# A block-product layer on one core: layer 2 of the step ahead in two parts, and the x sums after the gates' normalisation

## The reference

```python
def _moe_ref(x, w_gate, w1, w2):          # x: 1152 x 512, E = 8, F = 1024
    logits = x @ w_gate
    P = np.exp(logits - logits.max())
    for _ in range(8):                    # the gates' normalisation
        P /= P.sum(1, keepdims=True) + 1e-09
        P /= P.sum(0, keepdims=True) + 1e-09
        P *= N / E
    out = np.zeros((N, D), dtype=np.float32)
    for e in range(E):
        h = np.maximum(x @ w1[e], 0.0)
        ye = h @ w2[e]
        out += P[:, e:e + 1] * ye
    return out
```

## Time and profile before

| what | value |
|---|---|
| time, median of 3 runs | 1185.52 us (1184.65 to 1187.41) |
| profiled execution: its own time | 1187.6 us |
| profiled execution: span | 1185.8 us |
| PE busy | 1136.4 us (96%), 6974 instructions |
| DVE busy | 749.1 us (63%) |
| ACT busy | 442.9 us (37%) |
| POOL busy | 354.7 us (30%) |
| chain that ended last | PE 81%, DVE 6%, POOL 5%, issue 3%, ACT 3%, DMA 1% |
| mean granted clock of TensorE | 0.983 of full speed |

### The profile page before, as it was taken

The page is one execution under the profiler, slowest core; times in us unless marked ns, Lnnn a source line. Parts: engine busy times, 40 slices in busy tenths (PEclk is TensorE's granted clock), DMA queues, the critical chain, the costliest instruction groups (busy, mean ns, idle before and its releaser), DMA issues.

```text
span 1185.8 us, 19445 instructions
## 1 busy us (share of the span) xinstructions
PE 1136.4 (96%) x6974; PEld 1006.5 (85%) x6979; DVE 749.1 (63%) x1325; ACT 442.9 (37%) x936; POOL 354.7 (30%) x386
## 2 busy tenths in 40 slices
PE   7899798899999999999999999999997999999997
PEld 4678797789899898899888988999896889888885
DVE  5776834775775877776677587561136556665663
ACT  4772122433433443343443343241132334343332
POOL 3332706342333333243333244200001222222221
PEclk8899999999999999999999999999998999999999
DMA  7714001221321221231131121070003666655653
GB/s 177 185 39 147 29 1 53 78 66 36 107 72 36 72 90 51 74 90 36 54 102 48 48 71 36 15 269 28 28 18 112 177 186 179 177 145 162 177 143 80
DMA packets 120775, 109.52 MB, mean 92 GB/s; under 512 B 23712, under 2 KB 95392, under 8 KB 120704
## 3 DMA queue, kind: packets, MB, share of 16 engines
q1 hardware_dynamic: 113624, 93.53, 25.8%
q0 software_dynamic: 5904, 14.75, 5.9%
q10 hardware_dynamic: 1176, 0.30, 0.1%
HBM read 97.64 MB, written 10.91 MB: 92 GB/s over the span
## 4 chain that ended last, share of the span: by engine, by line
PE 81%; DVE 6%; POOL 5%; issue 3%; ACT 3%; DMA 1%; POOLq 0%; DVEq 0%; SPq 0%; ACTq 0%
PE bank L1657 7%; PE bank L1661 6%; PE bank L1659 6%; PE bank L1701 6%; PE bank L1702 6%; PE bank L1703 6%; PE bank L1517 6%; PE bank L1531 6%; PE bank L1518 6%; PE bank L1519 6%; PE bank L1533 6%; PE bank L1532 6%; DVE acc L1200 2%; POOL wopf L614 1%; ACT wop L862 1%
## 5 line engine op out<-in xcount | busy, mean ns | idle before, releaser
L1702 PE MATMUL bank<-w2lo,hS 128*128 128x512 f32 x432 | 168.5, 390 | 0.0
L1701 PE MATMUL bank<-w2hi,hS 128*128 128x512 f32 x432 | 168.5, 390 | 0.0
L1703 PE MATMUL bank<-w2hi,hS 128*128 128x512 f32 x432 | 168.2, 389 | 0.0
L622 POOL TENSOR_TENSOR s<-u,s 128x256 f32<-128x256 f32 (+1 forms) x48 | 38.7, 806 | 346.3 <-DVE u L1220 346.3
L1531 PE MATMUL bank<-w2hi,hhi 128*128 128x512 f32 (+1 forms) x336 | 132.9, 395 | 0.0
L1533 PE MATMUL bank<-w2hi,hlo 128*128 128x512 f32 (+1 forms) x336 | 131.4, 391 | 0.0
L1532 PE MATMUL bank<-w2lo,hhi 128*128 128x512 f32 (+1 forms) x336 | 131.3, 391 | 0.0
L1657 PE MATMUL bank<-xhi,wop 128*128 128x320 f32 (+1 forms) x384 | 115.8, 302 | 5.6 <-ACT s L881 5.6
L1659 PE MATMUL bank<-xlo,wop 128*128 128x320 f32 (+1 forms) x384 | 114.2, 297 | 0.0
L1661 PE MATMUL bank<-xhi,wop 128*128 128x320 f32 (+1 forms) x384 | 114.2, 297 | 0.0
L1025 DVE SCALAR_TENSOR_TENSOR hlo<-bank,hhi 128x336 fp32r<-128x336 f32 (+1 forms) x112 | 58.4, 523 | 70.9 <-ACT hhi L903 40.3
(11 more groups left out here) (259 smaller groups left out, 2759.0 us busy)
## 6 DMA issues: line engine op xcount, KB each, us to landing
w1p<-in_moe_w_dram SPq DMA_DIRECT2D x96, 256.0 KB, 3.5
w1raw<-in_moe_w_dram SPq DMA_DIRECT2D x44, 512.0 KB, 5.4
w2raw<-in_moe_w_dram SPq DMA_DIRECT2D x44, 512.0 KB, 5.4
w2p<-in_moe_w_dram SPq DMA_DIRECT2D x48, 256.0 KB, 2.9
qkraw<-in_q_dram SPq DMA_DIRECT2D x16, 144.0 KB
out_dram<-ysb POOLq DMA_DIRECT2D x3, 768.0 KB, 10.4
x1rows<-acc SPq DMA_DIRECT2D x9, 256.0 KB, 2.0
qkraw<-in_k_dram SPq DMA_DIRECT2D x14, 144.0 KB
```

What stands on the lines that cost most here:

```text
L1701: pe.matmul(y[:, :], hh, w2hi[:, f, :], start=(p == 0 and fi == 0), stop=False)
L1702: pe.matmul(y[:, :], hh, w2lo[:, f, :], start=False, stop=False)
L1703: ins = pe.matmul(y[:, :], hl, w2hi[:, f, :], start=False, stop=(p == POS - 1 and fi == 1))
```

## The change

It has four parts.

1. PE: `products` gets an argument `between`. Behind its third product (S1) PE now runs the first two row tiles of layer 2 of the step before (`FRONT`), and behind the seventh product the other two or three (`BEHIND`).
2. DVE: `weight_lo` is split into two functions, and both halves are for step j+1 instead of j+2. They, and `weight2_lo` (now of step j itself), move from the end of the step to the place between `u2` and `u3`. The additions into `acc` are made in two parts: the first two tiles before `u3`, the others at the end of the step. ACT's and POOL's order for the weights stays.
3. POOL starts `x_sums` only when the first tile of `acc` is written, which is behind the last round of the normalisation.
4. The last x sum of the second block moves: on POOL from before step (1, 0) to behind step (1, 2), on ACT and DVE to the end of step (1, 3), and PE waits for it before the last product of step (1, 4). POOL makes the weight sums of step (1, 0) ahead of the first block's last x sum.

```diff
@@ POOL
+            pool.wait_ge(acc_ready, 1)
             for b in range(2):
                 x_sums(b)
             pool.wait_ge(l1_done, G * FC)
+            weight_sums(1, 0)
             pool.wait_ge(xsum_lo, 6)
             x_last_sum(0)
-            for j in range(2):
-                weight_sums(1, j)
-            x_last_sum(1)
+            weight_sums(1, 1)
             step(1, 0)
             for e in range(1, LAST):
                 for j in range(1, STEPS):
                     step(e, j)
+                    if e == 1 and j == 2:
+                        x_last_sum(1)
                 step(e + 1, 0)
...
+        FRONT, BEHIND, WHOLE_STEP = slice(0, 2), slice(2, None), slice(0, None)
+        def step_tiles(b, part):
+            return range(BLOCKS[b][0] // P, sum(BLOCKS[b]) // P)[part]
@@ ACT, step
                 if (j + 1) % STEPS < POS and not (e == LAST and j == STEPS - 1):
                     weight2_hi(e + (j + 1) // STEPS, (j + 1) % STEPS)
+                if n == POS - 1:
+                    act.wait_ge(xsum_ready, 4)
+                    x_sum_hi(3, 1)
...
             expert(0, 1)
+            weight_hi(1, 0)
             act.wait_ge(xsum_ready, 3)
             x_sum_hi(3, 0)
-            for j in range(2):
-                weight_hi(1, j)
-            act.wait_ge(xsum_ready, 4)
-            x_sum_hi(3, 1)
+            weight_hi(1, 1)
             weight2_hi(1, 0)
             step(1, 0)
@@ DVE, step
                 dve.tensor_tensor(u2_, banks[1][:, 0:h], s1_, ALU.add).then_inc(u2_ready, 1)
+                if j < POS and not first:
+                    weight2_lo(e, j)
+                if not first and not (e == LAST and j == STEPS - 1):
+                    weight_lo(e + (j + 1) // STEPS, (j + 1) % STEPS)
+                    weight_sums_lo(e + (j + 1) // STEPS, (j + 1) % STEPS)
+                if j == POS:
+                    add_tiles(e, 0, FRONT)
+                if j == 0 and not first:
+                    add_tiles(e - 1, 1, FRONT)
                 dve.wait_ge(p7_added, n + 1)
...
                 low(3, s5_)
-                if ahead:
-                    weight_lo(e + (j + 2) // STEPS, (j + 2) % STEPS)
-                if (j + 1) % STEPS < POS and not (e == LAST and j == STEPS - 1):
-                    weight2_lo(e + (j + 1) // STEPS, (j + 1) % STEPS)
+                if n == POS - 1:
+                    x_sum_lo(3, 1)
                 if j == POS:
-                    add_block(e, 0)
+                    add_tiles(e, 0, BEHIND)
                 if j == 0 and not first:
-                    add_block(e - 1, 1)
+                    add_tiles(e - 1, 1, BEHIND)
@@ PE
                 product(S1, t1, banks[2], True, p5_in_bank)
+                if between is not None:
+                    second(*between, FRONT)
                 pe.wait_ge(s1_ready, n + 1)
...
+                if e == 1 and j == POS:
+                    pe.wait_ge(xsum_lo, 8)
                 product(A22, t4, banks[1], False, p4_added)
...
             products(1, 0)
-            pe.wait_ge(xsum_lo, 8)
             for e in range(1, LAST):
                 for j in range(STEPS):
-                    products(e + (j + 1) // STEPS, (j + 1) % STEPS)
-                    second(e, j)
-            for j in range(STEPS):
-                if j + 1 < STEPS:
-                    products(LAST, j + 1)
-                second(LAST, j)
+                    products(e + (j + 1) // STEPS, (j + 1) % STEPS, (e, j))
+                    second(e, j, BEHIND)
+            for j in range(STEPS - 1):
+                products(LAST, j + 1, (LAST, j))
+                second(LAST, j, BEHIND)
+            second(LAST, STEPS - 1)
```

More of the change, by code:

```diff
@@ L1184, in weight_lo, with weight_sums_lo @@
                                   ).then_inc(wop_lo, 1)
+            def weight_sums_lo(e, j):
+                n = e * STEPS + (j - STEPS)
+                hi, lo = (wop[:, j % 2, i, :, :, :] for i in range(2))
                 dve.wait_ge(wop_hi, 2 * n + 2)
@@ L1193, in weight2_lo, with add_tiles @@
                                   ).then_inc(w2s_lo, 1)
-            def add_block(e, b):
-                for i in range(BLOCKS[b][0] // P, sum(BLOCKS[b]) // P):
+            def add_tiles(e, b, part):
+                for i in step_tiles(b, part):
                     dve.wait_ge(l2_done, e * TILES + (i + 1))
@@ L1201, in add_block, with step @@
                                              ALU.mult, ALU.add).then_inc(acc_ready, 1)
-            def step(e, j, ahead=True):
+            def step(e, j):
                 n, h = e * STEPS + (j - STEPS), HALVES[j // POS]
@@ L1266, in group @@
                         if tt == 0:
+                            weight_lo(1, 0)
+                            weight_sums_lo(1, 0)
                             x_sum_lo(3, 0)
-                            weight_lo(1, 0)
                         if tt == 1:
                             weight_lo(1, 1)
-                            x_sum_lo(3, 1)
+                            weight_sums_lo(1, 1)
                     add_tile(e, g * TT + tt, plain)
@@ L1287, in _ @@
             for j in range(1, STEPS):
-                step(LAST, j, j + 2 < STEPS)
+                step(LAST, j)
                 if j == POS + 1:
@@ L1293, in _ @@
             x_back_low(1)
-            add_block(LAST, 1)
+            add_tiles(LAST, 1, WHOLE_STEP)
             for g in range(G):
@@ L1644, in _, with products @@
             group2(0, 0, 2)
-            def products(e, j):
+            def products(e, j, between=None):
                 n, b = e * STEPS + (j - STEPS), j // POS
@@ L1684, in products, with second @@
                     pe.wait_ge(xsum_lo, 7)
+                if e == 1 and j == POS:
+                    pe.wait_ge(xsum_lo, 8)
                 product(A22, t4, banks[1], False, p4_added)
-            def second(e, j):
+            def second(e, j, part=WHOLE_STEP):
                 n, b, p = e * STEPS + (j - STEPS), j // POS, j % POS
@@ L1705, in second @@
                         ins.then_inc(l2_done, 1)
-                if p < POS - 1:
+                if p < POS - 1 and part != FRONT:
                     ins.then_inc(step_done, 1)
```

## The result

The changed kernel takes 1170.0 us (median of 4 runs, 1167.1 to 1173.6); the kernel before, run beside it, takes 1186.5 us. The ratio is 0.9864, with a 95% interval of 0.9828 to 0.9899: 16 us faster. Run once more beside other experiments, the pair gave 1170.03 against 1185.83 us, ratio 0.9867 (0.985 to 0.9885). The forecast was 1169.6 us from 1185.5. The shortest of the four runs has a mean granted clock of 0.992 and the longest 0.986.

A forecast was written before the change was run, and what follows sets the result against it. PE, busy 96% of the span, was taken as the bound, so only its idle time and slow clock could be won. Terms -7.8 - 8.2 + 1.5 - 3.1 + 1.7 = -15.9 us took the median from 1185.5 to 1169.6 us; range 1164 to 1177.

The forecast's parts named there:

- Normalisation: Gate rounds, part 3: with POOL's x sums away, PE's two waits (6.2 us) and the slow clock go; gain 7.8 us.
- The 2 us of cover for ACT: Delayed x sums end near 162 us; ACT asks for the second block's first sum at 164.
- Start of the block products: First two product steps, part 4: 11.1 us of waits and slow clock shrink to 2.9; gain 8.2 us.
- The three waits: Step (1, 1): FRONT waits 0.9 us for low, A12 0.3 for s1, A22 1.7 for u3; 2.9 in all.
- The table of times in the prediction: Due and ready times for step (1, 1): A12 due at t + 5.9, s1 ready at t + 6.1 at the earliest.
- t: The end of a step's last product, from which the prediction counts times in us; 409.09 in the profile rows.
- The moved x sum: Step (1, 3): POOL's moved operations meet DVE's splits, 4.6 us in place of 3.1; loss 1.5 us, once.
- Settled steps: Waits for u2 go (6.8 us), short new waits for u3 come (3.7 us); net gain 3.1 us.
- The lower bound of this term: Settled steps: net gain of -2 us if u3 comes 0.5 us later in 16 steps.
- the mild rival: First block's steps: s1 or the splits 0.5 us later in 16 steps, 8 us, time 1177.6 us; chance 0.13.
- The end: Behind the last product, BEHIND covers only 4.1 us, so PE waits for low; loss 1.7 us.
- Late splits, `u3` in every step of the first block: Contended splits make u3 2.6 us later in 16 steps: +42 us, time 1211; chance 0.05.

The follow-up runs named there:

- part 3 alone: The kernel before, with only POOL's x sums started behind the first addition into acc: 1179.4 us, ratio 0.9946.
- part 4 alone: The kernel before, with only the last x sum moved, layer 2 and the splits staying: 1185.6 us, ratio 0.9988.
- The late restoring: The changed kernel, with POOL restoring x for the second block only when DVE's last low part is written: 1167.1 us (one run).
- the version with whole additions: The changed kernel with DVE's queue as before (splits for step j+2, then whole additions, at the step's end), layer 2 in two parts: 1229.8 us, ratio 1.0363.
- the version that differs in DVE's queue alone: The changed kernel with DVE's splits back at the end of the step, behind the second part of the additions, still in two parts: 1163.6 us, ratio 0.9811.

## Why the prediction was right

The time was 1170.0 for 1169.6, and the traces' three stretches changed by -15.6 us for -15.9. The terms, from PE's timeline, hold too, though two of them came out near by errors that cancel:

- **Normalisation:** -7.8 forecast, -8.3 in the trace; part 3 alone shows it by itself, with the clock. The 2 us of cover for ACT were 2.1.
- **Start of the block products:** -8.2 forecast, -7.9. The three waits were said to be 0.9, 0.3 and 1.7; PE's rows show 0.69 for `low`, less than 0.1 for `s1` (A12's first matmul starts 0.27 us behind the one before it, for 0.23), and 1.58 for `u3`, with a full clock. The text laid the gain to part 4, and the wait of 3.58 us for `s1` to queues standing before the last x sum. The runs correct that: with the sum moved that wait stayed at 3.6 us; part 4 alone wins 4.5 us there (5.7 with part 3), and the other 2.4 to 3.4 come with layer 2 between the products of step (1, 1), which puts PE's demand for `s1` off. The table of times in the prediction had this (A12 due at t + 5.9 with `FRONT`), the heading did not.
- **The moved x sum:** +1.5 forecast. In step (1, 3) the four products take 4.89 us for the 3.22 of other steps with j = 2 or 3: +1.67. The last two of POOL's three operations:

```profile
216.96 1.57 POOL L591 TENSOR_TENSOR xlof<-xlof,xlo 128x640 f32<-128x640 f32 x1
218.61 2.43 POOL L592 TENSOR_TENSOR xlof<-xlof,tB 128x640 f32<-128x640 f32 x1
```

DVE's first two splits beside them:

```profile
218.10 1.51 DVE L1206 TENSOR_TENSOR w2lo<-w2p,w2hi 128x1024 fp32r<-128x1024 f32 x1
219.53 2.32 DVE L1192 TENSOR_TENSOR wop<-w1p,wop 128x768 fp32r<-128x768 f32 x1
```

And PE's last product, which waits for `u3`:

```profile
223.38 0.39 PE L1679 MATMUL bank<-xhi,wop 128*128 128x256 f32 x1 [1.76 <-DVE u L1243]
```

  The 768 split, issued at 219.53, ends at 221.85, 0.81 behind POOL's operation (218.61 + 2.43 = 221.04); POOL's operation itself ends 1.43 behind DVE's split before it (218.10 + 1.51 = 219.61). They take turns here too. The rule of the Trainium skill (SBUF — State Buffer, Who interferes with whom) fits this trace; the price by it, 2.1, was 0.4 above the measured one. The sum's own price was near by luck: it had the three splits at 2.1, 1.4 and 1.1 us, and they took 1.51, 2.32 and 1.21 (0.08 of overlap at each not taken off). The end of POOL's second operation cost the first split 0.3, its third cost the 768 split 1.4, and the last split ran free.
- **Settled steps:** -3.1 forecast. It came to -3.0, by luck: the difference of two sizes was near, the sizes were not. The waits for `u2` were put at 6.8 us, PE's idle time as the view of waits counts it. By distances of starts the product step behind additions took 6.33 for 5.09 us (j = 1, five times), 6.61 for 6.15 (j = 5, five times) and once 7.30 for 6.15: 9.7 us. The new waits for `u3` were put at 0.2 and 0.3 us; they are 0.29 (j = 2, 3) and 0.45 (j = 0), 5.4 us with the first expert's in place of 3.7. The first error is one of reading: the view of waits starts an idle time at the modelled end of the last matmul, 0.16 us behind the time at which the next one could have started, and it doesn't count that the first matmul behind a wait takes 0.22 us to the next start in place of 0.12. That makes 0.26 us for each wait. The second is smaller: `u3` ended at t + 10.0 as forecast (307.79 - 297.78), but PE's next matmul started 0.06 us later still, and was such a slower first one. A product step before the change, from which the 9.7 is worked out:

```profile
306.93 0.28 PE L1657 MATMUL bank<-xhi,wop 128*128 128x256 f32 x1
...
313.26 0.39 PE L1701 MATMUL bank<-w2hi,hS 128*128 128x512 f32 x1
```

  Together with some 0.03 us in each step for the extra change between layer 2 and products, the steps won 3.0 us without the x sum (and 1.3 with it). The lower bound of this term was mis-summed: `u3` 0.5 us later in 16 steps is 8 us, as the mild rival has it, and 3.1 - 8 is -4.9, not -2.
- **The end:** +1.7 forecast, +1.8: 12.71 us for 48 layer-2 matmuls, which at 0.2275 are 10.92. The late restoring took exactly this away, so that the cause is shown.

Of the rivals, none came true in the changed kernel. Late splits, `u3` in every step of the first block, are real as a mechanism at j = 0, 2 and 3, at 0.3 to 0.45 us and not at 2.6. Waits that only move appear when the additions stay whole and behind the splits: that version is 43 us slower. The prediction did not see that the move of the splits was itself the cause of the new waits and could have been left out.

## What to carry to other kernels

When PE's work is moved ahead of a handshake, move only what is then late on the other engines: here the additions that free PE's banks, ahead of the weight splits, and not the splits, whose deadline had moved away by itself. Whether the additions also had to be made in two parts was not tested. Cut PE's timeline at fixed pieces of work and compare the distances of starts; the idle column misses about 0.26 us of each wait, which was 2.9 of 9.7 us here. Before a step is moved off one engine's queue, look at what the partner that shares its turn runs at the new place: DVE's gate operations, splits and `low` operations and POOL's x sums made each other up to 1.4 us slower where they met, in the normalisation, at the x sum and at the end. DVE's additions into `acc`, whose large input is a bank, were not slowed: three took 2.07 us with POOL's x sums beside them.

## What was not expected of the hardware

How a wait hits the clock is not read off its length alone. In the kernel before, a wait of 3.09 us left the clock at full speed. The next one of 3.10 us, 8 us later, was followed by matmuls of 384 columns that take 0.52 us each for 0.33 (0.32 for 0.17 by starts), with a granted clock of 0.50 from 141.4 to 144.8 us, the lower of its two levels. Two waits of 2.0 and 1.5 us within 5 us were followed by slow matmuls too (0.50 from 203.5 to 206.2 us), and the changed kernel's 0.7 and 1.6 within 7 us were not. In the version with whole additions every one of the 11 waits, 3.6 to 4.4 us each by PE's starts, was followed by slow matmuls. Its block products take 622.2 us for 553.3 in the version that differs in DVE's queue alone: 44.4 us are the waits and 24 the slow matmuls behind them, 2.2 us for each wait.
